# Transposes of the identity between the attention steps, before the first expert product

## The reference

```
scores = scale * np.matmul(q, k.transpose(0, 1, 3, 2))
keep = is_sink | in_window                 # 4 sink columns, a window of 128
a = softmax(np.where(keep, scores, -1e9))
attn_out = np.matmul(a, v)                 # 2 batches x 8 heads x 768 x 64
h = x @ w_in                               # 512 -> 2048
x = (np.maximum(h, 0) + alpha * np.minimum(h, 0)) @ w_out
# then: argmax routing of each token to one of 8 experts, at most 384 tokens
# each, relu(x @ w1[e]) @ w2[e], times the gate's probability
```

## Time and profile before

| what | value |
|---|---|
| median of 3 executions | 673.5 us |
| lowest and highest | 670.8 and 673.88 us |
| the profiled execution, its own time | 675.09 us |
| the profiled execution, from first to last instruction | 673.4 us |
| TensorE busy with matmuls | 601.2 us |
| VectorE, ScalarE, GpSimd busy | 372.2, 287.3, 159.0 us |
| TensorE busy in the first 60 us | 39.35 us |
| TensorE busy from 60 to 120 us | 57.65 us |

### The profile page before, as it was taken

The page is one execution under the profiler, slowest core; times in us unless marked ns, Lnnn a source line. Parts: engine busy times, 40 slices in busy tenths (PEclk is TensorE's granted clock), DMA queues, the critical chain, the costliest instruction groups (busy, mean ns, idle before and its releaser), DMA issues.

```text
span 673.4 us, 11546 instructions
## 1 busy us (share of the span) xinstructions
PE 601.2 (89%) x3759; PEld 503.2 (75%) x3759; DVE 372.2 (55%) x1133; ACT 287.3 (43%) x681; POOL 159.0 (24%) x213
## 2 busy tenths in 40 slices
PE   4678989999999999999999999929999789859993
PEld 3457878888888888888888899728877667647772
DVE  4545777667567656665664455372853644664410
ACT  4644555433344334333432211233864655664520
POOL 5543222222232222222221000031121322330112
PEclk9999999999999999999999999958999898989997
DMA  7520533201020102010000400294875666865100
GB/s 205 142 80 17 157 82 93 64 17 33 18 63 17 32 17 64 17 33 17 33 17 1 157 1 1 68 290 158 273 244 171 212 214 192 288 212 191 63 32 18
DMA packets 73394, 67.36 MB, mean 100 GB/s; under 512 B 43013, under 2 KB 49173, under 8 KB 73329
## 3 DMA queue, kind: packets, MB, share of 16 engines
q1 hardware_dynamic: 69488, 57.76, 27.7%
q0 software_dynamic: 3840, 8.77, 4.5%
HBM read 57.75 MB, written 12.58 MB: 104 GB/s over the span
## 4 chain that ended last, share of the span: by engine, by line
PE 82%; DVE 5%; ACT 4%; issue 4%; DMA 1%; POOL 1%; ACTq 0%; DVEq 0%; POOLq 0%
PE bank L805 21%; PE bank L807 20%; PE bank L806 20%; PE bank L800 9%; PE bank L842 4%; PE bank L868 4%; PE bank L936 2%; ACT fw L639 1%; DMA fw<-y_scratch,v_or_route 1%; DVE rw L1299 1%; ACT wh L618 1%; DVE wl L1076 1%; PE bank L882 1%; DMA o_sb<-in_q_dram 0%; ACT rw L760 0%
## 5 line engine op out<-in xcount | busy, mean ns | idle before, releaser
L805 PE MATMUL bank<-wh,rw 128*128 128x512 f32 x416 | 170.9, 411 | 10.6 <-issue 3.5
L806 PE MATMUL bank<-wl,rw 128*128 128x512 f32 x416 | 165.2, 397 | 0.0
L807 PE MATMUL bank<-wh,rw 128*128 128x512 f32 x416 | 165.1, 397 | 0.0
L1076 DVE TENSOR_TENSOR wl<-fw,wh 128x512 fp32r<-128x512 f32 x160 | 100.2, 685 | 38.0 <-ACT wh L618 36.7
L805 PE MATMUL bank<-rw,wh 128*128 128x256 f32 x384 | 113.2, 295 | 0.0
L807 PE MATMUL bank<-rw,wl 128*128 128x256 f32 x384 | 109.0, 284 | 0.0
L806 PE MATMUL bank<-rw,wh 128*128 128x256 f32 x384 | 108.7, 283 | 0.0
L720 ACT CAST rw<-fw 128x256 fp32r<-128x256 f32 x96 | 39.0, 406 | 151.1 <-DVE fw L1253 151.0
L805 PEld LDWEIGHTS bank<-wh,rw 128*128 128x128 f32 x416 | 80.1, 193 | 28.3 <-issue 10.2
L807 PEld LDWEIGHTS bank<-wh,rw 128*128 128x128 f32 x416 | 79.5, 191 | 17.9
L618 ACT CAST wh<-fw 128x512 fp32r<-128x512 f32 x160 | 88.0, 619 | 6.0 <-DMA fw<-in_moe_w_dram 2.7
(11 more groups left out here) (138 smaller groups left out, 654.1 us busy)
## 6 DMA issues: line engine op xcount, KB each, us to landing
fw<-in_moe_w_dram SPq DMA_DIRECT2D x128, 256.0 KB, 4.8
fw<-in_moe_w_in_dram SPq DMA_DIRECT2D x16, 256.0 KB, 3.1
fw<-in_moe_w_out_dram SPq DMA_DIRECT2D x16, 256.0 KB, 2.8
o_sb<-in_q_dram SPq DMA_DIRECT2D x12, 256.0 KB, 3.2
o_sb<-in_k_dram SPq DMA_DIRECT2D x12, 256.0 KB, 3.9
y_scratch<-fw SPq DMA_DIRECT2D x12, 256.0 KB, 2.1
out_dram<-v_or_route SPq DMA_DIRECT2D x12, 256.0 KB, 2.9
v_raw<-in_v_dram SPq DMA_DIRECT2D x11, 256.0 KB, 3.3
```

What stands on the lines that cost most here:

```text
L805: pe.matmul(dst, ah, bh, start=start, stop=False, skip_group_check=True)
L806: pe.matmul(dst, ah, bl, start=False, stop=False, skip_group_check=True)
L807: return pe.matmul(dst, al, bh, start=False, stop=stop, skip_group_check=True)
L1076: dve.tensor_tensor(wl[:, hf, col:col + PIECE], staged, f32(wh[:, hf, col:col + PIECE]), ALU.subtract).then_inc(weights_low_split, 1)
```

## The change

A new helper on TensorE issues k transposes of the identity into the second bank of `H_BANK`. No one reads them, and they wait for nothing of their own. Ten stand ahead of the first transposes of q, seven behind those of k, and nine at the end of the attention part of each even step of the opening. These are 11 steps (n = 0, 2, ..., 20), so 99 transposes, and 116 with those of the start. The other engines' instructions and all waits stay.

```diff
+            def keep_busy(k):
+
+                for _ in range(k):
+                    tr(H_BANK[1][:, 0:P], ident[:, :])
+
...
             pe.wait_ge(constants_made, 2)
 
+            keep_busy(10)
             q_T(0)
             k_T(0)
+            keep_busy(7)
...
                 if t is not None:
                     sink_values(t)
+                if n < OPEN:
+                    keep_busy(9 if n % 2 == 0 else 0)
                 if mh:
                     hidden(m + 1, 0)
```

## The result

The changed kernel takes 665.63 us (median of 4 executions, 664.13 to 666.3) where the kernel before takes 673.69 beside it: ratio 0.987, 95% interval 0.9837 to 0.9903. The forecast was 663.6, in a range of 658.5 to 671. The profiled execution of the changed kernel took 664.13 us.

What follows compares the result with a forecast made beforehand. The prediction took the opening to be a chain across engines whose TensorE blocks ran at 1.2 GHz. Eleven terms of time saved at 2.4 GHz sum to 9.85 us, which from the median of 673.5 gives 663.6 us, range 658.5 to 671.

Steps and rivals of the forecast that it cites:

- the clock doesn't rise on transposes: Opening: transposes leave the clock low and the steps' nine take 1.9 us each; 7.2 us slower, 680.7; chance 0.12.
- Which then holds: Opening: after rising between 5 and 9 us, the clock stays high through pauses, the longest 2.21 us.
- the second rival: Opening: the clock rises late or falls back; if up only at the third tile, 671 us; chance 0.07.
- Terms 4 and 5: Scores of pair 6 and four transposes, from 29.17: 0.95 us; values, scores, `p_T` from 34.20: 1.4 us saved.
- terms 1 and 2: Scores of pair 0: 0.4 us; `p_T` of pair 1 and q, k of tile 1 at 18.25: 0.35 us saved.
- 3: Scores of pair 4 and two transposes: 0.7 us saved at the high clock.
- 6: q and k of tile 2: they shrink by 0.9 us, of which 0.55 us counts as saved.
- 7 and 8: Scores and `p_T` of step 16: 0.95 us; values, scores, `p_T` from 44.20: 1.0 us, limited by ACT and DVE.
- 9: Scores and `p_T` of step 20: 0.95 us saved at the high clock.
- 10: Values, scores, `p_T` of step 22, up to the start of the product at 57.59: 1.2 us saved.
- 11: First product's 12 matmuls, the transposes of tile 3 and the second product: together 1.4 us saved.
- Step 8: Values, scores, `p_T` from 44.20, 1.0 us saved; its sign: pair 10's exponentials follow DVE rather than the copy.

Runs made afterwards that it cites:

- the early v: Changed kernel with the load of v for tiles 3 and later issued one step earlier, ahead of that step's weight pieces: 664.78 us, 0.9845 of the kernel before.

## Why the prediction was right

**The state of the clock** was read rightly from durations against the column, and *whether it rises* too: it rose about 7 us, in the bounds of 5 to 9, on transposes alone. The rival "the clock doesn't rise on transposes" is refuted by the scores at 7.56 us in the trace of the changed kernel, 0.62 us instead of 1.02. The Trainium skill (TensorE: Matmul & The Clock Gate, "Part 4: PE-mode transpose") says that the full clock does not engage for transposes; for these of float32 the same row shows that it does.

**"Which then holds" was wrong.** I took the 2.21 us as the longest pause and compared it with one of 6 us. A row that the prediction itself uses spoke against that: at 555.59 eight transposes took 1.94 us, at the low clock, behind a pause of 2.14 us, and the four ahead of that pause, at 552.85, had taken 0.60, at the high one. So the clock had fallen behind a pause shorter than 2.21 us. The clock fell behind a pause of 1.79 us, with little work on either side, in both profiled executions of the changed kernel, at once in one and 1.7 us later in the other. This is part of the second rival, which had 0.07. The prediction named a fall between 30 and 50 us as a sign that it is wrong; the low stretch, 27.5 to 34.3, began before and reached into it, while the first product, at 50.93, kept within the 53 that it allowed. The pause is not the whole cause: with the steps' transposes alone and with the early v the clock passed it and fell at 34 us. In the three kernels with 14 in that pause, and in that with eighteen a step, it did not fall before 50 us. Terms 4 and 5 (0.95 and 1.4) gave 0.01 and 0.55 for it. With the pause filled they gave 0.86 (34.20 − 31.87 less 1.47 ahead at the scores) and 1.26 (38.08 − 34.49 less 2.33).

**The other terms** held within 0.15 us each: 0.37 and 0.5 for terms 1 and 2 (0.4, 0.35), 0.61 for 3 (0.7), 0.69 for 6 (0.55), 1.88 for 7 and 8 (1.95), 0.85 for 9 (0.95), 1.2 for 10 (1.2), 1.35 for 11 (1.4). Step 8 showed its sign: the exponentials that stood at 47.84 start at 43.20, and on the chain they follow DVE's mask at 42.74 instead of the copy (they belong to pair 9; the prediction calls them pair 10's). Where the clock held through the opening the sum came to 9.55 us, against 9.85.

**The cost of the transposes** was read rightly: 1.15 us for nine with the modelled end, 0.98 from 16.90 to the next block, hidden in the copy of the probabilities. What they cost uncovered is shown by eighteen.

**"Later stages keep their high clock" was wrong** in one place: TensorE waits for v of tile 3 in both kernels, but in the changed kernel's first profile the clock fell there as well, which cost 1.4 us. The kernel before had kept it in its first profile:

```profile
89.56 0.44 PE L868 MATMUL bank<-fw,v_or_route 128*64 128x128 f32 x4 [2.33 <-issue]
...
90.14 0.63 PE L842 MATMUL bank<-rw 64*128 64x260 f32 x6
```

It fell there in five more of the kernels, and in the repeated kernel before. Whether it does depends on the execution.

**The sum and its luck.** The forecast took 9.85 us off, and the medians differ by 8.1. The opening gave 8.0 of them in the profiled execution, behind v of tile 3 only 6.75 were left, and at the end it was 11. So the opening is explained by its terms, and how close the median came owes something to falls in later stages that differ from one execution to the next and that the prediction took as equal.

## What to carry to other kernels

Check the clock by the duration of one shape in two places before believing a column, and look for the first place of dense work: what lies ahead of it on the critical chain may be running at half speed. Work that no one reads, put in pauses that another engine sets, can buy that clock. Here it paid most where it was about as long as the pause: 17 in front bought nothing by themselves, four a step about half, and eighteen lay 3.5 us on the opening's chain. A wait is worth removing twice where the clock falls behind it: that for v cost 2.14 us and the fall 1.4.

## What the runs showed of the hardware

- Transposes of 128x128 alone, 25 of them, raised TensorE's clock between 1.59 and 7.56 us; where the added ones were of 16x16, the scores still took 1.02 us up to those at 35.23.
- The clock fell behind pauses of 1.79 us (27.69) and 2.14 us (81.46), where the kernel before had kept it through 2.33 us at the same wait, and it was low for 6.8 and 3.4 us. Elsewhere it stayed low for longer: 10.2 us (27.8 to 38) with four a step, 37 us with the start alone.
- The same program has its falls at different moments in different executions: 27.5 and 29.2 us in two profiles of the changed kernel, at v of tile 3 in one of them only.
